# The order of the gate and value products in a fused attention and two-layer MLP kernel

## The reference

```
qn, kn = q, k scaled to unit norm over the 6016 rows
a   = softmax(kn^T qn / tau)            # 256 x 256
x   = v @ a                             # 6016 x 256
# layer 1 (RMS norm, SiLU gate)
xn  = x / rms(x) * rms_g
x   = (silu(xn @ w_gate) * (xn @ w_val)) @ w_out      # 256 -> 1536 -> 256
# layer 2 (sigmoid gate, no norm, its own weights)
out = (sigmoid(x @ w_gate) * (x @ w_val)) @ w_out
```

## Time and profile before

| | us |
|---|---|
| median of 3 runs | 1280.36 (1279.92 to 1280.54) |
| the profiled execution | 1280.59 |
| its span, first to last instruction | 1278.8 |
| PE busy | 1266.5 (99%), 5711 matmuls |
| PEld busy | 1063.9 (83%), 5711 loads |
| DVE busy | 655.2 (51%) |
| ACT busy | 454.5 (36%) |
| POOL busy | 37.7 (3%) |
| granted TensorE clock, mean | 1.000 |

### The profile page before, as it was taken

One profiled execution on the slowest core, in us unless ns is written; L12 is line 12 of the kernel. 1 busy time (PEld: TensorE's weight loads), 2 busy tenths in 40 slices (PEclk: granted clock), 3 DMA queues, 4 the chain that ended last, 5 costly groups with the idle time before them and its releaser, 6 DMA issues.

```text
span 1278.8 us, 15529 instructions
## 1 busy us (share of the span) xinstructions
PE 1266.5 (99%) x5711; PEld 1063.9 (83%) x5711; DVE 655.2 (51%) x1014; ACT 454.5 (36%) x737; POOL 37.7 (3%) x32
## 2 busy tenths in 40 slices
PE   8999999999999999999999999999999999999998
PEld 7878888888888888888888888888888888889888
DVE  6776544544554554554454455455455455446343
ACT  5443533333333333333333333333333333333332
POOL 0000600000000000000000000000000000000000
PEclk9999999999999999999999999999999999999999
DMA  9920000100100100010010010010010001000000
GB/s 342 307 84 1 1 1 1 34 0 0 33 0 0 33 0 0 6 27 0 0 33 0 0 33 0 0 33 0 0 29 4 0 0 29 1 1 18 1 17 13
DMA packets 60569, 34.43 MB, mean 27 GB/s; under 512 B 50816, under 2 KB 54144, under 8 KB 60544
## 3 DMA queue, kind: packets, MB, share of 16 engines
q1 hardware_dynamic: 60544, 34.09, 9.3%
HBM read 27.92 MB, written 6.16 MB: 27 GB/s over the span
## 4 chain that ended last, share of the span: by engine, by line
PE 98%; DMA 1%; DVE 0%; SPq 0%; POOL 0%; issue 0%; DVEq 0%
PE ps L662 21%; PE ps L664 21%; PE ps L663 21%; PE ps L783 10%; PE ps L782 10%; PE ps L781 10%; PE ps L728 3%; PE ps L688 1%; PE ps L704 1%; DMA qk<-in_k 1%; PE ps L697 0%; SPq L251 0%; POOL small L297 0%; PE ps L714 0%; DVE w_lo_v L443 0%
## 5 line engine op out<-in xcount | busy, mean ns | idle before, releaser
L597 DVE TENSOR_TENSOR h<-ps,h 128x512 f32<-128x512 f32 (+1 forms) x288 | 196.0, 681 | 309.9 <-PE ps L664 296.0
L391 ACT ACTIVATE h_hi<-h 128x512 fp32r<-128x512 f32 (+1 forms) x288 | 179.5, 623 | 396.1 <-DVE h L597 394.5
L385 ACT ACTIVATE h<-ps 128x512 f32<-128x512 f32 (+1 forms) x288 | 169.7, 589 | 384.6 <-PE ps L664 384.4
L602 DVE TENSOR_TENSOR h_lo<-h,h_hi 128x512 fp32r<-128x512 f32 (+1 forms) x288 | 195.4, 678 | 130.9 <-ACT h_hi L391 127.1
L783 PE MATMUL ps<-h_hi,w_lo_o 128*128 128x512 f32 (+1 forms) x576 | 222.9, 387 | 0.0
L781 PE MATMUL ps<-h_hi,w_hi_o 128*128 128x512 f32 (+1 forms) x576 | 222.9, 387 | 0.0
L782 PE MATMUL ps<-h_lo,w_hi_o 128*128 128x512 f32 (+1 forms) x576 | 222.8, 387 | 0.0
L593 DVE TENSOR_TENSOR h<-ps,h 128x512 f32<-128x512 f32 (+1 forms) x144 | 98.0, 680 | 154.2 <-ACT h L385 154.1
L781 PEld LDWEIGHTS ps<-h_hi,w_hi_o 128*128 128x128 f32 x576 | 109.8, 191 | 20.7
L783 PEld LDWEIGHTS ps<-h_hi,w_lo_o 128*128 128x128 f32 x576 | 109.7, 190 | 20.9
L782 PEld LDWEIGHTS ps<-h_lo,w_hi_o 128*128 128x128 f32 x576 | 109.7, 190 | 20.3
(11 more groups left out here) (111 smaller groups left out, 1320.1 us busy)
## 6 DMA issues: line engine op xcount, KB each, us to landing
v_in<-in_v SPq DMA_DIRECT2D x44, 128.0 KB, 2.9
out<-out_sb SPq DMA_DIRECT2D x44, 128.0 KB, 2.4
qk<-in_q SPq DMA_DIRECT2D x10, 512.0 KB, 7.2
qk<-in_k SPq DMA_DIRECT2D x10, 512.0 KB, 9.6
w_raw_g<-in_moe_w_gate SPq DMA_DIRECT2D x6, 512.0 KB, 7.6
w_raw_v<-in_moe_w_val SPq DMA_DIRECT2D x6, 512.0 KB, 8.4
w_raw_o<-in_moe_w_out SPq DMA_DIRECT2D x6, 512.0 KB, 9.3
qk<-in_q SPq DMA_DIRECT2D x3, 256.0 KB, 3.1
```

The lines of the kernel that those rows point to most:

```text
L385: nc.scalar.activation(h[:, slot, 0:w], ps[:, GATE[slot], 0:w], ACT.Sigmoid).then_inc(sig_done, 1)
L391: nc.scalar.activation(h_hi[:, part, 0:w], h[:, slot, 0:w], ACT.Copy).then_inc(hi_done, 1)
L597: nc.vector.tensor_tensor(h[:, slot, 0:w], ps[:, VALUE[slot], 0:w], h[:, slot, 0:w], ALU.mult).then_inc(h_done, 1)
L602: nc.vector.tensor_tensor(h_lo[:, part, 0:w], h[:, slot, 0:w], h_hi[:, part, 0:w].bitcast(F32), ALU.subtract).then_inc(lo_done, 1)
```

## The change

`up` no longer finishes the gate before it begins the value. For each chunk it issues six products that go to the gate bank and the value bank in turn: high weights by high x for gate and value, low weights by high x for both, high weights by low x for both. The moving operand is then the same for four products in a row, and the PSUM bank changes with each. The 12 matmuls, their 12 weight loads, their operands and their sums are the same set as before. The gate's last matmul is now the 11th of the tile and not the 6th; the value's last is the 12th, as before. The wait for the x parts of chunk 1 comes after 6 matmuls in place of 3.

```diff
-                for name, bank, done in (("g", GATE, gate_done), ("v", VALUE, value_done)):
-                    wh, wl = w_hi[name + layer], w_lo[name + layer]
-                    three(ps[:, bank[slot], 0:w],
-                          [(wh[:, c, j * P:(j + 1) * P], wl[:, c, j * P:(j + 1) * P], x[0][:, c, 0:w],
-                            x[1][:, c, 0:w]) for c in range(CC)],
-                          parts_of_x if name == "g" else None).then_inc(done, 1)
+                gate, value = ps[:, GATE[slot], 0:w], ps[:, VALUE[slot], 0:w]
+                for c in range(CC):
+                    if parts_of_x:
+                        parts_of_x(c)
+                    first, last = c == 0, c == CC - 1
+                    (g_hi, v_hi), (g_lo, v_lo) = ([t[n + layer][:, c, j * P:(j + 1) * P] for n in "gv"]
+                                                  for t in (w_hi, w_lo))
+                    x_hi, x_lo = x[0][:, c, 0:w], x[1][:, c, 0:w]
+                    nc.tensor.matmul(gate, g_hi, x_hi, start=first, stop=False)
+                    nc.tensor.matmul(value, v_hi, x_hi, start=first, stop=False)
+                    nc.tensor.matmul(gate, g_lo, x_hi, start=False, stop=False)
+                    nc.tensor.matmul(value, v_lo, x_hi, start=False, stop=False)
+                    gate_mm = nc.tensor.matmul(gate, g_hi, x_lo, start=False, stop=last)
+                    value_mm = nc.tensor.matmul(value, v_hi, x_lo, start=False, stop=last)
+                gate_mm.then_inc(gate_done, 1)
+                value_mm.then_inc(value_done, 1)
```

## The result

The changed kernel takes 1290.61 us (median of 4 runs, 1290.31 to 1291.01) against 1280.14 before: a ratio of 1.0082, 95% interval 1.0067 to 1.0097. It is slower by 10.5 us, where 8.6 were forecast. The profiled execution has a span of 1289.2 us against 1278.8.

What follows compares the result with a forecast made beforehand. PE's matmuls laid end to end bound the kernel (98% of the span). Pace 0 plus late-gate waits 5.85 + 0.73 + 0.13 + 0.55 + 1.05 (tile 4 weights) + 0.28 = 8.6 us gave 1289.0 us, 0.7% slower; range 1282 to 1294.

Steps and rivals of the forecast that it cites:

- The pace: Matmuls in `up`: a kept operand earns nothing and a changed bank costs nothing, taken as 0 over 2304 steps.
- Rivals A and B: A: kept operand pays, -30 us, about 1259, chance 0.06; B: new order slows pace, +13 us, about 1302, chance 0.08.
- The shift: Gate's sigmoid starts 1.13 us later; in layer 1, 512 wide, line 597 and all behind it is 1.05 late.
- The covered waits: PE's waits for h_lo (8.2 us after the value) and for the banks (5.4 us) stay covered, costing nothing.
- the end: Last tile: h_lo is done just before `down` starts, slack already gone, so 0.28 us comes on top.
- The turns: `down` waiting for DVE's transposes of Y: nine at 0.65, 5.85 us; last block 0.73 (layer 1) and 0.13 (layer 2).
- The restart: Extra cost when PE resumes after a late release: 0.15 us each, read from the one wait before.
- The copies of block 1: Copies of Y in layer 1 of block 1: shift 1.05, slack 0.65, so 0.40 + 0.15 = 0.55 us.
- X is ready in time at every pass: The later wait for chunk 1 of x saves nothing, since x is always ready; counted as no time.
- Rival C: Turns of Y hide the shift in DVE's idle time, leaving 1.9 us, about 1282.3; chance 0.08.
- Rival D: Clock swings to its lower level, about 6 us per hundredth of the span, some 1310 or more; chance 0.02.

## Why the prediction was right

- The pace. Taken as 0 from one step inside `down` that keeps its operand and changes its bank. Read to 0.01 us, one step is thin ground: over 2304 steps that is 23 us. The result bears it out: twelve products still take 2.72 us, and the runs with the operand kept, with the alternation at equal lateness, and with lateness alone leave nothing for it. Rivals A and B fall: neither the +13 us drawn from the warm-up nor the -30 drawn from rows 5 shows. What makes the steps of those two stages longer and shorter no run tells; the products of rows 5 are those of q and k (line 728), which the prediction wrongly calls the norm stage.
- The shift. 5 products late, less the 0.08 that line 597 had waited: the run with the increment alone moved has the same ten waits, and line 597 stands 0.73 behind line 593.
- The covered waits. The deadlines of `down` on h and of `up` on its banks were costed at nothing, by 36 and 24 products of lead. No wait of PE for either is listed; the only late h_lo is that of the end, which the sum had counted.
- The turns. Right in number (nine, and two of the last block) and in the 0.50 by which the release is late (0.49). The restart was mis-sized: taken as 0.15 from the one wait in the trace before, it is 0.23 at a turn. There the second product comes 0.46 after the end of the transposes (649.85 to 650.31), and after line 443 it was 0.38. That makes 0.08 a turn, and with some hundredths in the steps behind it 0.9 of the 1.4 us missing from the forecast. The copies of block 1 restart in the same way: they end at 133.15 and the second product comes at 133.60, 0.45 later, which is 0.22 for the restart. Why a wait for line 459 or 361 restarts more slowly than one for line 443 no run tells. All misses of the table lie on one side; none cancels another.
- "X is ready in time at every pass" failed once. Ahead of the first product of block 1 the second layer 1 pass waits for DVE's line 525, which the late gate pushed from 119.74 to 122.31, 1.0 more than PE itself was late by then. The first of its two instructions ends at 122.99, 0.11 before the product is due at 122.87 + 0.23 = 123.10. No wait is listed for it, but the weight load comes late, and so do the products behind it:

```profile
122.31 1.28 DVE L525 TENSOR_TENSOR xs_lo<-x_raw,xs_hi 128x512 fp32r<-128x512 f32 x2
...
122.87 0.39 PE L793 MATMUL ps<-h_hi,w_lo_o 128*128 128x512 f32 x1
123.11 0.19 PEld L760 LDWEIGHTS ps<-xs_hi,w_hi_g 128*128 128x128 f32 x1 [0.28 <-issue]
123.14 0.47 PE L760 MATMUL ps<-xs_hi,w_hi_g 128*128 128x512 f32 x1
...
123.45 0.40 PE L761 MATMUL ps<-xs_hi,w_hi_v 128*128 128x512 f32 x1
```

- Rival C, that DVE's idle time takes the shift up, falls by the rows of the turn above: from the sigmoid to the transposes each step of the chain starts within 0.04 of the end of the one before, so each hands the shift on.
- Rival D, the clock. The granted clock is 1.00 over the run: with a change of bank at each of 3456 products it stays at its upper level, and twelve products keep their 2.72 us. The longest wait in the stream is 1.7 us. The Trainium skill (TensorE: Matmul & The Clock Gate, § A second HAM failure mode: psum-queue depth-cycling) tells of a kernel whose clock swings because it cycles through PSUM banks and idles between its groups; here the banks change without idle time between the groups, and no swing shows. The rival's price of 1310 or more follows from no row.

## What to carry to other kernels

The end of an accumulation is a release, and the order of the products decides when it comes: finishing two results together takes from the first one the cover that the second one's products gave it. To price such a change, read for every wait of the bounding engine how early its releaser is; what costs is not the shift but the shift less the slack. The edge isn't sharp: here a release 0.16 us ahead of its use still cost 0.08, while one 0.30 ahead (in the kernel before, the last block's layer 2) cost nothing. Where neither operand nor bank moves the pace of the bounding engine, look for the time in the few waits and in the layout of the weights, not in which operand stays.

## What the runs showed of the hardware that was not expected

- A late release costs more than its lateness: 0.15 us behind one releaser (line 443) and 0.22 to 0.23 behind others (lines 361 and 459), and 0.08 is lost even when the release comes 0.16 ahead of the matmul.
- A single weight load that reads every second number lengthens three steps, by 0.013 us in all; six in a row cost 0.047 together, 0.008 each.
- In the profiled executions of the run with the increment on the 11th matmul and of the run with the high weights half by half, the products of q and k ran for a stretch at a granted clock of 0.62 on average (so partly at 1.2 GHz and not 2.4), behind waits of 2.46 and 2.11 us for a load, and came 0.43 apart and not 0.22. Each lost about 1.6 us by it. In the changed kernel that wait was 1.76 and in the kernel before 1.54, and the clock stayed at 1.00. Both executions with the low stretch have the old order of products, so it isn't the work of the alternation. The windows' columns are length, busy us by engine, clock, DMA; two rows of the first run, then one of the second:

```profile
10.00:14.50 4.50, 3.76 (x10) 3.07 (x11) 1.81 (x2) 3.15 (x2) 0.00 (x0) 0.62 0.96 368
14.50:20.00 5.50, 5.50 (x28) 5.00 (x27) 5.22 (x5) 2.59 (x2) 0.00 (x0) 1.00 0.93 372
...
10.00:14.50 4.50, 4.31 (x12) 3.58 (x13) 2.35 (x2) 3.69 (x2) 0.00 (x0) 0.62 0.97 358
```
